# Adding the softmax guard on VectorE instead of ScalarE in a fused attention and mixture-of-experts kernel

## The chip, the cores and the metric

The kernel runs on one core of one Trainium2 chip. The core has TensorE (PE in the profile) for matrix products, VectorE (DVE), ScalarE (ACT) and GpSimd (POOL) for elementwise work, SyncE (SP) and several DMA queues for transfers. The engines run side by side and meet at semaphores: an instruction waits until a counter has reached a value, and raises another one when it is done. The metric is the device time of one execution, in microseconds.

## The reference

Three layers follow one another: attention with rotary embedding, a top-1 mixture of experts, and a dense layer with a tanh. The change lies in attention alone, in the sum that the softmax divides by:

```python
def _attn_ref(q, k, v):                       # (4, 8, 576, 64)
    q_rot, k_rot = (rotate(q), rotate(k))
    scores = scale * np.matmul(q_rot, k_rot.transpose(0, 1, 3, 2))
    scores = scores - np.max(scores, axis=-1, keepdims=True)
    attn = np.exp(scores)
    attn = attn / (np.sum(attn, axis=-1, keepdims=True) + 1e-09)
    return np.matmul(attn, v).astype(np.float32)
```

What comes after it is `_moe_ref` (2304 tokens, 8 experts) and `_moe2_ref` (`g = h - tanh(h)` between two products).

## The kernel before, in words

Attention takes the 32 heads in 16 pairs, 0 to 15. A pair has nine tiles of scores: four of each head with 128 query rows, and one mixed tile of the 64 rows left over from both. The body of pair p runs nine steps, i = 0 to 8, on every engine at once. In a step TensorE computes the scores of tile i of the next pair, p + 1 (L373), transposes a slice of the exponentials of pair p (L420) and multiplies transposed slices with the values (L441, L444, L447). VectorE takes the maximum of the new score tile (`maximum`, L617). ScalarE computes its exponential and the row sums (`exp`, L517). Each transposed slice is then split into a rounded high part, by ScalarE (`round_hi`, L538, `pt_hi`), and the remainder, by VectorE (`split_lo`, L633, `pt_lo`). TensorE multiplies both. So each slice goes TensorE, ScalarE, VectorE, TensorE. The transposed slices of a pair have names; the one of the mixed tile, split in step 5, is M, and the first product that needs both parts of M is that of `values(..., "MA")`, whose first instruction is L441.

GpSimd prepares later pairs: it splits the values (`split_v`, L312 and L317), multiplies the raw q and k with the cosines and sines (`rope`, L338 and L339) and adds and splits the result (`add_up`, L323, L326, L332). These are seven elementwise instructions for each pair, up to pair 12's body. Before the first of them it waits until TensorE is done with the values of the pair before (`pv_done`). SyncE starts the transfers that stack q and k (L184 to L193).

Once a pair, 1e-9 is added to the nine row sums, and the reciprocal is taken. The first is `guard` on ScalarE in step 3 (L548), the second `invert` on VectorE in step 5 (L638). `normalise` uses the reciprocals in the next body. The row sums were finished one body earlier, as `exp` works a pair ahead.

The order on each engine is written out by hand: an engine takes its instructions in the order of the program. Pairs 4 to 13 run on VectorE in a hardware loop, the others are written out; there a semaphore's value has to be computed in a register first.

Of the kernel before, what the change touches and what calls it, by code (L numbers as in the profile page):

```python
# [11 lines left out]
ALU = mybir.AluOpType  # L12
ACT = mybir.ActivationFunctionType
AX = mybir.AxisListType

P = 128
# [26 lines left out]
def attention(nc, qk, v, cos, sin, ident, fold, emb_t, route_consts, x_all, lg_all, tail_dram,  # L43
# [7 lines left out]
    with ExitStack() as ctx:  # L51
        def sb(name, shape, dt=F32):
            return ctx.enter_context(nc.sbuf_tensor(name, shape, dt))

        def sem(name):
            return ctx.enter_context(nc.semaphore(name))
# [3 lines left out]
        TILES = 2 * FULL + 1  # L60
# [26 lines left out]
        neg_max = [sb(f"neg_max{r}", [P, TILES]) for r in range(2)]  # L87
        row_sum = [sb(f"row_sum{r}", [P, TILES]) for r in range(2)]
        guarded = sb("guarded", [P, TILES])
        tiny = sb("tiny", [P, 1])  # L90
        inv_sum = [sb(f"inv_sum{r}", [P, TILES]) for r in range(2)]
        probs = [sb(f"probs{r}", [P, FULL, 2 * S]) for r in range(2)]
        probs_mix = [sb(f"probs_mix{r}", [P, S]) for r in range(2)]
# [28 lines left out]
        zero_set = sem("zero_set")  # L122
# [14 lines left out]
        exp_done = sem("exp_done")  # L137
# [3 lines left out]
        pv_done = sem("pv_done")  # L141
        o_evac = sem("o_evac")
        fold_ready = sem("fold_ready")
        guard_done = sem("guard_done")
        norm_step = sem("norm_step")
        x_done = sem("x_done")
        tail_stored = [sem(f"tail_stored{r}") for r in range(2)]
# [7 lines left out]
        def block_of(i):  # L155

            return i if i < MIX else i - MIX - 1
# [6 lines left out]
        def _(sp):  # L164
# [89 lines left out]

            body(0, 0, first=True)

            sp.wait_ge(zero_set, 2)
            body(1, 1, clears=True)
            with sp.Fori(1, PAIRS // 2 - 2) as m:
                for r in range(2):  # L260
# [249 lines left out]
        @block.scalar  # L510
        def _(act):
            def exp(p, r, i):

                act.wait_ge(max_done, p * TILES + i + 1)
                at = int(i > MIX) * S
                dst = probs_mix[r][:] if i == MIX else probs[r][:, block_of(i), at:at + S]
                nc.scalar.activation(dst, score[(r + i) % 2], ACT.Exp, bias=neg_max[r][:, i:i + 1],  # L517
                                     accum_out=row_sum[r][:, i:i + 1]).then_inc(exp_done, 1)

            def round_hi(p, r, name, first=False):  # L520
                if name[0] == "B":

                    act.wait_ge(pv_done, p * VALUES + VALUE["A" + name[1]] + 1)
                elif not first:
                    last = {"X": "B3", "M": "MB", "C": "MB"}[name] if name in "XMC" else "B" + name[1]

                    act.wait_ge(pv_done, (p - 1) * VALUES + VALUE[last] + 1)

                act.wait_ge(pt_ready, p * UNITS + UNIT[name] + 1)
                src = turned[SLOT[name]]  # L530
                if name == "X":
                    op = nc.scalar.activation(ends[:, 0:FULL, :, 0, :],
                                              src.rearrange("p (k u s) -> p k u s", u=2, s=TAIL), ACT.Identity)
                elif name == "C":
                    op = nc.scalar.activation(ends[:, FULL, :, 0, :], corner.rearrange("p (u s) -> p u s", u=2),
                                              ACT.Identity)
                else:
                    op = nc.scalar.activation(pt_hi[:, FULL if name == "M" else int(name[1]), P:P + MAIN], src,  # L538
                                              ACT.Identity)
                op.then_inc(hi_done, 1)  # L540

            def guard(p, r, first=False):

                act.wait_ge(exp_done, (p + 1) * TILES)
                if not first:

                    act.wait_ge(norm_step, p)
                nc.scalar.activation(guarded[:], row_sum[r][:], ACT.Identity, bias=tiny[:]).then_inc(guard_done, 1)  # L548

            def evac(p, u, first=False):  # L550

                act.wait_ge(pv_done, p * VALUES + VALUE["MB" if u else "MA"] + 1)
                if not first:

                    act.wait_ge(fold_ready, p * 2)
                nc.scalar.activation(out_t[:, u, :], acc, ACT.Identity)
                nc.scalar.activation(out_tail[:, :, u, :], acc_tail[u].rearrange("p (h s) -> p h s", h=2),
                                     ACT.Identity).then_inc(o_evac, 1)

            def body(p, r, first=False, second=False, last=False):  # L560
                for i in range(TILES):
                    round_hi(p, r, STEPS[i][0], first)
                    if i == 1 and not first:
                        evac(p - 1, 1, second)
                    if i == 3:
                        guard(p, r, first)
                    if i == 6:
                        evac(p, 0, first)
                    if not last:
                        exp(p + 1, 1 - r, i)  # L570
                    for name in STEPS[i][1:]:
                        round_hi(p, r, name, first)

            act.dma_start(cos_sb[:, 1, :], cos).then_inc(tables_in, 16)
            act.dma_start(sin_sb[:, 1, :], sin).then_inc(tables_in, 16)
            act.dma_start(id_sb[:], ident).then_inc(consts_in, 16)
            act.dma_start(fold_sb[:, :, E:E + DH], fold.rearrange("p (g d) -> p g d", g=PB)).then_inc(consts_in, 16)
            for u in range(2):
                for w in range(2):
                    act.dma_start(fold_sb[u * DH:(u + 1) * DH, :, w * FW:w * FW + E],  # L580
                                  emb_t.rearrange("(g w d) e -> w d g e", w=2, d=DH)[w]).then_inc(consts_in, 16)

            act.wait_ge(zero_set, 2)
            act.wait_ge(tables_in, 32)
            for table in (cos_sb, sin_sb):
                nc.scalar.activation(table[:, 0, :], table[:, 1, :], ACT.Copy, scale=SCALE).then_inc(table_scaled, 1)
            for i in range(TILES):
                exp(0, 0, i)
            body(0, 0, first=True)
            body(1, 1, second=True)  # L590
            with act.Fori(1, PAIRS // 2 - 1) as m:
                for r in range(2):
                    body(m * 2 + r, r)
            body(PAIRS - 2, 0)
            body(PAIRS - 1, 1, last=True)
            evac(PAIRS - 1, 1)

        @block.vector
        def _(dve):
# [34 lines left out]

            def invert(p, r):

                dve.wait_ge(guard_done, p + 1)
                nc.vector.reciprocal(inv_sum[r][:], guarded[:]).then_inc(norm_step, 1)  # L638

            def normalise(p, r, u, stores=None):  # L640

                dve.wait_ge(norm_step, p + 1)

                dve.wait_ge(fold_ready, p * 2 + u + 1)
                at = u * (MIX + 1)
                by = inv_sum[r][:, at:at + FULL].unsqueeze(2)
                batch, h = p // PB, (p % PB) * 2 + u
                x_at, l_at = E * (1 - u), DH * u
                nc.vector.tensor_tensor(lg_all[:, bass.ds(batch * FULL, FULL), bass.ds(h * E, E)],
                                        folded[1 - u][:, :, l_at:l_at + E], by.to_broadcast([P, FULL, E]), ALU.mult)  # L650
                op = nc.vector.tensor_tensor(x_all[:, bass.ds(batch * FULL, FULL), bass.ds(h * DH, DH)],
                                             folded[1 - u][:, :, x_at:x_at + DH], by.to_broadcast([P, FULL, DH]), ALU.mult)
                if u:
                    if stores is not None:

                        dve.wait_ge(tail_stored[r], stores)
                    op = nc.vector.tensor_tensor(tail_sb[r][:], folded_mix,
                                                 inv_sum[r][:, MIX:MIX + 1].to_broadcast([P, FP]), ALU.mult)
                op.then_inc(x_done, 1)
# [11 lines left out]
                    if i == 3 and not first:  # L671
                        normalise(p - 1, 1 - r, 1, stores)

            nc.vector.memset(tiny[:], 1e-9).then_inc(zero_set, 1)
            nc.vector.memset(zeros[:], 0.0).then_inc(zero_set, 1)
            dve.wait_ge(tables_in, 32)
            rope_first(1, first_k_in, first_k_mult, first_k_done)

# [15 lines left out]
            body(PAIRS - 2, 0, stores=(PAIRS // 2 - 2) * 32)  # L694
            body(PAIRS - 1, 1, last=True, stores=(PAIRS // 2 - 1) * 32)
            normalise(PAIRS - 1, 1, 0)
            normalise(PAIRS - 1, 1, 1, (PAIRS // 2 - 1) * 32)

# [1022 lines left out]
```

## Time and profile before

| | us |
|---|---|
| median of 3 runs | 1111.47 |
| lowest and highest | 1110.96, 1112.81 |
| the profiled execution: its own time | 1110.96 |
| its span in the trace | 1109.1 |
| PE busy | 985.1 (89%) |
| DVE busy | 595.5 (54%) |
| ACT busy | 582.4 (53%) |
| POOL busy | 415.7 (37%) |

Busy times are sums over the whole span, and the stages differ: attention takes the first 350 us or so, and POOL has work mostly there and in the expert layer. An engine can be busy half of the time and still be waited for at one place in each step. A row of the timeline gives an instruction's start and duration in us, and in brackets how long its engine had been idle before it and what ended that.

### The profile page before, as it was taken

How to read it: one execution, taken by the hardware profiler on the slowest of the kernel's cores; microseconds unless marked ns; L12 is line 12 of the kernel's file. 1: busy time of each engine (PE TensorE's matmuls, PEld its weight loads, DVE VectorE, ACT ScalarE, POOL GpSimd, SP SyncE). 2: the span in 40 equal slices, each digit the busy share in tenths (PEclk: the TensorE clock that was granted, in tenths of full speed). 3: DMA queues.
4: the chain of work that ended last, by engine and by line, in shares of the span. 5: the costliest groups of instructions: out<-in, count | busy, mean ns of one | idle time of the engine just before them, and what ended most of it. 6: DMA issues, size and time to landing. Idle time of an engine off the chain costs nothing. (4 is left out here: it accounts for less than half of the span.)

```text
span 1109.1 us, 18954 instructions
## 1 busy us (share of the span) xinstructions
PE 985.1 (89%) x5604; PEld 871.1 (79%) x5605; DVE 595.5 (54%) x1195; ACT 582.4 (53%) x1273; POOL 415.7 (37%) x246
## 2 busy tenths in 40 slices
PE   1899999999995039999999976999999999999996
PEld 1899899989984038888888855888989889899895
DVE  4677777777773731111111104777666666666764
ACT  1677777777772632222322214666565565655653
POOL 3998788887510428309948305000000000000000
PEclk9999999999998569999999997999999999999999
DMA  8777777767503455314433106111000000000001
GB/s 236 192 207 197 219 189 202 206 186 205 145 21 90 169 188 202 97 47 151 152 123 113 38 30 200 58 48 48 1 19 10 0 28 0 13 15 0 28 2 28
DMA packets 63077, 113.82 MB, mean 103 GB/s; under 512 B 20032, under 2 KB 24640, under 8 KB 61120
## 3 DMA queue, kind: packets, MB, share of 16 engines
q1 hardware_dynamic: 52352, 92.62, 29.0%
q10 hardware_dynamic: 7808, 11.31, 3.2%
q0 software_dynamic: 2880, 9.44, 2.5%
q8 instruction: 18, 0.29, 0.1%
q14 instruction: 19, 0.16, 0.1%
HBM read 60.58 MB, written 24.41 MB: 77 GB/s over the span
## 5 line engine op out<-in xcount | busy, mean ns | idle before, releaser
L1429 PE MATMUL hd_ps<-y_hi,w_hi 128*128 128x384 f32 x384 | 130.9, 341 | 7.8 <-DVE g_sb L1599 7.8
L1429 PE MATMUL hd_ps<-y_lo,w_hi 128*128 128x384 f32 x384 | 129.6, 338 | 0.0
L1429 PE MATMUL hd_ps<-y_hi,w_lo 128*128 128x384 f32 x384 | 129.3, 337 | 0.0
L1499 ACT ACTIVATE mag<-hd_ps 128x384 f32<-128x384 f32 x96 | 47.3, 493 | 152.2 <-PE hd_ps L1429 149.8
L617 DVE TENSOR_REDUCE neg_max<-ps 128x1 f32<-128x576 f32 x144 | 108.1, 751 | 31.4 <-PE ps L373 28.9
L633 DVE TENSOR_TENSOR pt_lo<-ps,pt_hi 128x512 fp32r<-128x512 f32 x144 | 99.2, 690 | 43.3 <-ACT pt_hi L538 41.7
L538 ACT ACTIVATE pt_hi<-ps 128x512 fp32r<-128x512 f32 x144 | 86.8, 604 | 58.9 <-PE ps L420 57.5
L1447 PE MATMUL o_ps<-w_hi,g_hi 128*128 128x512 f32 x288 | 115.0, 399 | 2.2 <-DVE g_lo L1608 2.2
L1447 PE MATMUL o_ps<-w_hi,g_lo 128*128 128x512 f32 x288 | 114.3, 397 | 0.0
L1608 DVE TENSOR_TENSOR g_lo<-g_sb,g_hi 128x384 fp32r<-128x384 f32 x96 | 53.5, 558 | 112.3 <-ACT g_hi L1514 112.3
L1447 PE MATMUL o_ps<-w_lo,g_hi 128*128 128x512 f32 x288 | 113.5, 394 | 0.0
L517 ACT ACTIVATE probs<-ps,neg_max 128x576 f32<-128x576 f32 x128 | 95.5, 746 | 26.0 <-DVE neg_max L617 25.7
L420 PE MATMUL ps<-id_sb,probs 128*128 128x128 f32 x576 | 87.8, 279 | 5.4 <-DVE pt_lo L633 5.0
L1102 POOL TENSOR_TENSOR w_hi<-w_stage,one 128x1024 f32 (+1 forms) x32 | 60.6, 1894 | 79.4 <-ACT h_row L1205 59.8
L444 PE MATMUL ps<-pt_hi,v_split 128*128 128x256 f32 (+1 forms) x320 | 85.5, 348 | 1.9 <-issue 0.5
L1429 PEld LDWEIGHTS hd_ps<-y_hi,w_hi 128*128 128x128 f32 x384 | 72.5, 189 | 16.3 <-DVE g_sb L1599 12.9
L373 PE MATMUL ps<-k_hh,q_st 128*128 128x288 f32 x256 | 59.2, 315 | 25.0 <-DMA q_st<-qk_lo 23.1
L1275 DVE TENSOR_TENSOR h_lo<-ht_ps,h_hi 128x512 fp32r<-128x512 f32 x40 | 25.8, 686 | 98.3 <-ACT h_hi L1230 98.3
L1106 POOL TENSOR_TENSOR w_lo<-w_stage,w_hi 128x1024 f32 (+1 forms) x32 | 76.7, 2396 | 4.6 <-POOL w_hi L1102 4.0
L420 PEld LDWEIGHTS ps<-id_sb,probs 128*128 128x128 f32 x576 | 67.7, 142 | 11.2 <-DVE pt_lo L633 9.4
L1429 PEld LDWEIGHTS hd_ps<-y_lo,w_hi 128*128 128x128 f32 x384 | 72.5, 189 | 3.1
L1268 DVE TENSOR_TENSOR x_lo<-xt_ps,x_hi 128x512 fp32r<-128x512 f32 x20 | 13.8, 692 | 110.7 <-ACT x_hi L1213 110.7
(208 smaller groups left out, 2429.8 us busy)
## 6 DMA issues: line engine op xcount, KB each, us to landing
w_stage<-in_w SPq DMA_DIRECT2D x32, 512.0 KB, 3.6
raw_qk<-in_qk SPq DMA_DIRECT2D x14, 1152.0 KB, 6.1
k_hh<-qk_hi SPq DMA_DIRECT2D x64, 144.0 KB, 2.8
k_ll<-qk_lo SPq DMA_DIRECT2D x64, 144.0 KB, 2.9
sorted_rows<-zeros SPq DMA_DIRECT2D x28, 256.0 KB, 6.2
x_row<-sorted_rows ACTq DMA_DIRECT2D x20, 256.0 KB, 2.7
y_rows<-y_row ACTq DMA_DIRECT2D x20, 256.0 KB, 2.1
q_st<-qk_hi SPq DMA_DIRECT2D x32, 144.0 KB, 3.0
```

What stands on the lines that cost most here:

```text
L373: last = nc.tensor.matmul(dst[:, a:z], q_st[r][u][:, at:at + P], keys[r][u][:, key:key + z - a], start=h == 0, stop=h == 1)
L420: last = nc.tensor.transpose(dst[:, j * P:(j + 1) * P], probs[r][:, j, key:key + P], id_sb[:])
L444: nc.tensor.matmul(ps[:, CUT - MAIN // 2 - P + a:CUT - MAIN // 2 - P + z], main, pt_hi[:, k, a:z], start=begin, stop=False)
L517: nc.scalar.activation(dst, score[(r + i) % 2], ACT.Exp, bias=neg_max[r][:, i:i + 1], accum_out=row_sum[r][:, i:i + 1]).then_inc(exp_done, 1)
L538: op = nc.scalar.activation(pt_hi[:, FULL if name == "M" else int(name[1]), P:P + MAIN], src, ACT.Identity)
L617: nc.vector.tensor_reduce(neg_max[r][:, i:i + 1], score[(r + i) % 2], AX.X, ALU.max, negate=True).then_inc(max_done, 1)
L633: nc.vector.tensor_tensor(lo_at, src, hi_at.bitcast(F32), ALU.subtract).then_inc(lo_done, 1)
L1102: nc.gpsimd.tensor_tensor(chunk_of(w_hi, slot, c), stage[:, c % RING, :], one[:].to_broadcast([P, CHUNK]), ALU.mult).then_inc(w_hi_done, 1)
L1106: nc.gpsimd.tensor_tensor(chunk_of(w_lo, slot, c), stage[:, c % RING, :], chunk_of(w_hi, slot, c).bitcast(F32), ALU.subtract).then_inc(w_s ...
L1429: op = nc.tensor.matmul(hd_ps[f % 2][:, 0:G], w[:, c, cols], y[:, c, :], start=c == 0 and h == 0, stop=c == DC - 1 and h == 2)
L1447: op = nc.tensor.matmul(o_ps[:, i, :], a[f % 2][:, rows], w[:, f, :], start=f == 0 and h == 0, stop=f == KF - 1 and h == 2)
L1608: nc.vector.tensor_tensor(g_lo[f % 2][:], g_sb[f % 2][:], g_hi[f % 2][:].bitcast(F32), ALU.subtract).then_inc(glo_done, 1)
```

## The change

The addition of 1e-9 moves from ScalarE to VectorE. The function `guard` is gone, with its semaphore `guard_done`. In `invert` a `tensor_tensor` now adds `row_sum` and `tiny`, and the reciprocal follows behind a wait for it; `norm_step` now goes up twice a pair. `tiny` grows from one column to nine, since it is now a tensor operand of its own and no longer a bias. ScalarE no longer waits for `zero_set` at the start, which now counts to 1.

```diff
-        tiny = sb("tiny", [P, 1])
+        tiny = sb("tiny", [P, TILES])
...
-            sp.wait_ge(zero_set, 2)
+            sp.wait_ge(zero_set, 1)
...
-            def guard(p, r, first=False):
-
-                act.wait_ge(exp_done, (p + 1) * TILES)
-                if not first:
-
-                    act.wait_ge(norm_step, p)
-                nc.scalar.activation(guarded[:], row_sum[r][:], ACT.Identity, bias=tiny[:]).then_inc(guard_done, 1)
-
...
-                    if i == 3:
-                        guard(p, r, first)
...
-            act.wait_ge(zero_set, 2)
             act.wait_ge(tables_in, 32)
...
             def invert(p, r):
 
-                dve.wait_ge(guard_done, p + 1)
+                dve.wait_ge(exp_done, (p + 1) * TILES)
+                nc.vector.tensor_tensor(guarded[:], row_sum[r][:], tiny[:], ALU.add).then_inc(norm_step, 1)
+                dve.wait_ge(norm_step, p * 2 + 1)
                 nc.vector.reciprocal(inv_sum[r][:], guarded[:]).then_inc(norm_step, 1)
 
             def normalise(p, r, u, stores=None):
 
-                dve.wait_ge(norm_step, p + 1)
+                dve.wait_ge(norm_step, p * 2 + 2)
...
-            nc.vector.memset(tiny[:], 1e-9).then_inc(zero_set, 1)
+            nc.vector.memset(tiny[:], 1e-9)
             nc.vector.memset(zeros[:], 0.0).then_inc(zero_set, 1)
+            dve.wait_ge(zero_set, 1)
             dve.wait_ge(tables_in, 32)
```

VectorE in step 5 of the loop's first pair, before. The `neg_max` rows are `maximum`, the `pt_lo` rows `split_lo`; the first `pt_lo` is slice A3 of step 4, the second is M.

```order
L633 TENSOR_TENSOR pt_lo<-ps,pt_hi 128x512 [waits hi_done]
L616 REGISTER_ALU
L617 TENSOR_REDUCE neg_max1<-ps 128x1 [waits scores_ready]
L638 RECIPROCAL inv_sum0<-guarded 128x9 [waits guard_done]
L622 REGISTER_ALU
L633 TENSOR_TENSOR pt_lo<-ps,pt_hi 128x512 [waits hi_done]
```

The same place after the change:

```order
L621 TENSOR_TENSOR pt_lo<-ps,pt_hi 128x512 [waits hi_done]
L604 REGISTER_ALU
L605 TENSOR_REDUCE neg_max1<-ps 128x1 [waits scores_ready]
L626 TENSOR_TENSOR guarded<-row_sum0,tiny 128x9 [waits exp_done]
L627 ISA
L628 RECIPROCAL inv_sum0<-guarded 128x9 [waits norm_step]
L610 REGISTER_ALU
L621 TENSOR_TENSOR pt_lo<-ps,pt_hi 128x512 [waits hi_done]
```

The addition, a register instruction (ISA) and a wait for the addition stand between the maximum of step 5 and the split of M.

ScalarE in step 3 of the same pair, before. The `pt_hi` rows are `round_hi`, the `probs1` row is `exp`.

```order
L538 ACTIVATE pt_hi<-ps 128x512 [waits pt_ready]
L548 ACTIVATE guarded<-row_sum0,tiny 128x9 [waits norm_step,exp_done]
L514 REGISTER_ALU
L517 ACTIVATE probs1,row_sum1<-ps,neg_max1 128x576 [waits max_done]
L529 REGISTER_ALU [waits pv_done]
L535 ACTIVATE pt_hi<-ps 128x2x64 [waits pt_ready]
```

The same place after the change:

```order
L537 ACTIVATE pt_hi<-ps 128x512 [waits pt_ready]
L513 REGISTER_ALU
L516 ACTIVATE probs1,row_sum1<-ps,neg_max1 128x576 [waits max_done]
L528 REGISTER_ALU [waits pv_done]
L534 ACTIVATE pt_hi<-ps 128x2x64 [waits pt_ready]
```

The exponential now follows the rounding directly. On TensorE, GpSimd and SyncE no instruction is added, taken away or moved.

## Rows read from the trace of the kernel before

**Rows 1.** Busy time of each engine in the body of pair 5, us.
```profile
136.00:155.50 19.50, 18.89 (x145) 17.51 (x145) 14.62 (x28) 14.16 (x35) 16.22 (x7) 1.00 0.71 195
```
**Rows 2.** Waits, first 430 us: total us, times, longest us.
```profile
PEld ps L420 <- DVE pt_lo L633: 9.4, 20, 0.6
```
**Rows 3.** Timeline, steps 5 to 7 of pair 5.
```profile
145.43 0.75 DVE L617 TENSOR_REDUCE neg_max<-ps 128x1 f32<-128x576 f32 x1
...
145.69 0.60 ACT L538 ACTIVATE pt_hi<-ps 128x512 fp32r<-128x512 f32 x1 [0.18 <-PE ps L420]
...
146.10 0.20 DVE L638 RECIPROCAL inv_sum<-guarded 128x9 f32<-128x9 f32 x1
...
146.32 0.69 DVE L633 TENSOR_TENSOR pt_lo<-ps,pt_hi 128x512 fp32r<-128x512 f32 x1
...
146.61 0.49 PEld L420 LDWEIGHTS ps<-id_sb,probs 128*128 128x128 f32 x4
...
147.07 0.19 PEld L441 LDWEIGHTS ps<-pt_hi,v_split 128*128 128x128 f32 x1
...
148.03 0.60 ACT L556 ACTIVATE out_t<-ps 128x512 f32<-128x512 f32 x1
```
**Rows 4.** Timeline of ScalarE, step 3 of pair 5.
```profile
140.85 0.29 ACT L548 ACTIVATE guarded<-row_sum,tiny 128x9 f32<-128x9 f32 x1
...
141.04 0.73 ACT L517 ACTIVATE probs<-ps,neg_max 128x576 f32<-128x576 f32 x1
...
142.54 0.28 ACT L535 ACTIVATE pt_hi<-ps 128x128 fp32r<-128x128 f32 x1 [0.68 <-PE ps L412]
```
**Rows 5.** Timeline, GpSimd around `invert`: pair 5, then pairs 2, 11, 12.
```profile
146.03 2.67 POOL L323 TENSOR_TENSOR rotated<-by_cos,by_sin 128x1152 f32<-128x1152 f32 x1
...
148.65 2.66 POOL L326 TENSOR_TENSOR qk_hi<-by_cos,by_sin 128x1152 fp32r<-128x1152 f32 x1
...
87.66 2.67 POOL L323 TENSOR_TENSOR rotated<-by_cos,by_sin 128x1152 f32<-128x1152 f32 x1
...
87.80 0.20 DVE L638 RECIPROCAL inv_sum<-guarded 128x9 f32<-128x9 f32 x1
...
262.30 2.68 POOL L323 TENSOR_TENSOR rotated<-by_cos,by_sin 128x1152 f32<-128x1152 f32 x1
...
262.34 0.20 DVE L638 RECIPROCAL inv_sum<-guarded 128x9 f32<-128x9 f32 x1
...
281.60 2.68 POOL L323 TENSOR_TENSOR rotated<-by_cos,by_sin 128x1152 f32<-128x1152 f32 x1
...
281.77 0.20 DVE L638 RECIPROCAL inv_sum<-guarded 128x9 f32<-128x9 f32 x1
```
**Rows 6.** Timeline, GpSimd around `invert` in pair 0.
```profile
47.00 2.67 POOL L338 TENSOR_TENSOR by_cos<-raw_qk,cos_sb 128x1152 f32<-128x1152 f32 x1
...
49.28 0.20 DVE L638 RECIPROCAL inv_sum<-guarded 128x9 f32<-128x9 f32 x1
```
**Rows 7.** Timeline of VectorE, two small additions or products, the second dependent.
```profile
360.55 0.17 DVE L888 TENSOR_TENSOR emb_n<-emb_n 128x8 f32<-128x8 f32 x1
360.75 0.17 DVE L889 TENSOR_TENSOR emb_n<-emb_n 128x8 f32<-128x8 f32 x1
```
**Rows 8.** Timeline of the routing stage, VectorE and GpSimd.
```profile
384.35 1.23 DVE L1001 TENSOR_TENSOR w_lo<-w_stage,w_hi 128x1024 f32 x1 [0.76 <-ACT w_hi L859]
...
384.72 1.68 POOL L832 DMA_INDIRECT sorted_rows<-token_rows,pos_i  x1 [0.30 <-issue]
...
389.46 1.27 DVE L1001 TENSOR_TENSOR w_lo<-w_stage,w_hi 128x1024 f32 x1 [1.12 <-ACT w_hi L859]
...
389.47 0.96 POOL L832 DMA_INDIRECT sorted_rows<-token_rows,pos_i  x1 [0.31 <-issue]
```
**Rows 9.** Timeline of the start, VectorE and SyncE's queue.
```profile
13.91 0.76 DVE L611 TENSOR_TENSOR qk_lo<-probs,qk_hi 128x576 fp32r<-128x576 f32 x1
...
15.32 1.30 SPq L193 DMA_DIRECT2D q_st<-qk_hi  x2
```

More of the change, by code:

```diff
@@ L143, in attention @@
         fold_ready = sem("fold_ready")
-        guard_done = sem("guard_done")
         norm_step = sem("norm_step")
```

## The prediction

> **What bounds the kernel now.** I read the busy times by stretch first. The body of pair 5 is a fair sample of attention: in 19.50 us TensorE is busy for 18.89, VectorE 14.62, ScalarE 14.16 and GpSimd 16.22, at a granted clock of 1.00 [rows 1]. TensorE sets the pace, the others have 3 to 5 us of slack each on average. That average hides how the engines meet, so the waits come next: TensorE's weight loads of the transposes wait for VectorE's `pt_lo` 20 times, 9.4 us in all and never more than 0.6 [rows 2]. TensorE therefore does wait for VectorE at times. The last view, the timeline around `invert`, shows how tight it is at the very place of the change [rows 3]. ScalarE's high part of M ends at 145.69 + 0.60 = 146.29, and VectorE's split of M starts at 146.32, 0.03 later. The split ends at 147.01, and TensorE's first load of `values("MA")` starts at 147.07. The load before it, a group of four, began at 146.61 and ran 0.49, to 147.10, with a little overlap as usual, so TensorE arrives there at the same moment. The slack between this split and TensorE is about 0.01 us. VectorE itself arrives a bit early: the reciprocal starts at 146.10 and overlaps its successor, as the maximum (145.43 + 0.75 = 146.18) overlapped the reciprocal by 0.08, so the split could start at 146.22 and waits 0.10 for ScalarE.
>
> Hence a delay d of VectorE between the maximum of step 5 and the split of M costs d - 0.10 - 0.01 there. It isn't made up later in the body: ScalarE's `evac` at 148.03 [rows 3] waits for the product with M, and the exponential and the roundings behind it on ScalarE move with it, and TensorE waits for those roundings' slices.
>
> **The change part by part.** *ScalarE loses the guard.* It starts at 140.85, and the exponential behind it at 141.04: the guard holds ScalarE's queue for 0.19 us, 16 times, 3.0 us in all [rows 4]. Behind that exponential ScalarE is idle for 0.68 us until TensorE has transposed the small corner [rows 4]. The 0.19 us only lengthens that idle time. Value: 0; if the cover were gone, a gain of 3.0.
>
> *The start.* ScalarE no longer waits for two memsets that were over long before, and its table load stands ahead of the wait for the tables. Even if this lets VectorE finish q earlier, SyncE starts q's stacking at 15.32, while VectorE's last part is done at 13.91 + 0.76 = 14.67 [rows 9]: SyncE is 0.65 us late by itself, busy with k's eight transfers. Value: 0, for `zero_set`, the wider `tiny` and VectorE's wait for its own memset too. If the cover were gone it would be some tenths once, either way.
>
> *VectorE gains an addition and a wait for it,* while nothing else stands in the way. A small `tensor_tensor` takes 0.17 us, and one that depends on it starts 0.20 after it [rows 7]. So the reciprocal starts 0.20 later than now, and the split can follow at 0.20 + 0.20 - 0.08 = 0.32 after the addition's start, where now it follows at 0.22 [rows 3]. That is 0.10 a pair, less 0.01 slack. In the loop a register instruction is added, which may cost up to another 0.1 or nothing. This hits 15 pairs (in pair 15 no scores are computed and VectorE has slack): 1.4 us, between 0 and 3.
>
> *The addition meets GpSimd.* It is the first VectorE instruction inside attention's steady state that reads two SBUF tensors (`row_sum` and `tiny`); the maxima read PSUM alone, `split_lo` and `normalise` PSUM and one SBUF tensor, the reciprocal one. At this moment GpSimd is in a long instruction that reads SBUF. In pair 5 its L323 started at 146.03, 0.07 us ahead of VectorE at 146.10, and the next one, L326, starts at 148.65 [rows 3, 5]. It is so in each of the eleven pairs 2 to 12: L323 starts 0.14 ahead in pair 2, 0.04 in pair 11, the closest, and 0.17 in pair 12 [rows 5]. The distance is stable because both engines follow TensorE's `pv_done` of the same product by fixed chains.
>
> Whether the two can read at once, the trace of before shows only from the side. In the routing stage VectorE runs a subtraction of two SBUF tensors from 384.35 to 385.58. GpSimd's indirect DMA issued at 384.72 takes 1.68 us, where the one at 389.47 takes 0.96 [rows 8]. It is longer by 0.72, nearly the 0.86 us for which VectorE's subtraction was still running: it waited for it. At 389.46 both start within 0.01; GpSimd takes its usual time and VectorE 1.27 instead of 1.23 [rows 8]. So there is something that one has to give up before the other gets it, and whoever comes second waits. The other order, VectorE behind a long elementwise GpSimd instruction, appears nowhere. Its bounds: 0.04 us (the one time VectorE was stretched) and the remainder of GpSimd's instruction, or that and one more. I take the remainder, as the row where one came clearly second waited for nearly all of it. L323 lasts until the next instruction at +2.62, less the 0.11 that VectorE comes behind on average over the eleven pairs: a wait of 2.51. With the 0.10 from above and the 0.01 of slack it is 2.60 a pair, 28.6 us for eleven.
>
> The Trainium skill says this outright ("SBUF — State Buffer", section "Who interferes with whom"): a VectorE instruction with two SBUF inputs contends with a GpSimd instruction that reads SBUF, and the one that comes second waits until the first has ended. By that rule the sum is the one that I make here; by the stretched row of VectorE alone it would be 0.04 a pair, some 2 us in all. Of the direction that counts, VectorE behind GpSimd's elementwise work, no row here speaks.
>
> *The other pairs.* In pair 0 GpSimd's L338 runs until 49.67 and VectorE comes at 49.28 [rows 6]: 0.39 + 0.09, about 0.5. In pair 1 GpSimd isn't tied to TensorE yet and both have been shifted by pair 0; anything from 0.1 to 2.7, and I take 0.5, as in pair 0. In pairs 13 and 14 GpSimd has no work left: 0.1 each. Pair 15: 0. Together 1.2.
>
> *Knock-on.* GpSimd has 3.3 us of idle time a pair [rows 1], and a longer body gives it more room. TensorE idles for 2.5 us in 22, at a clock of 1.00 now; I price no loss of clock.
>
> **Sum.** 28.6 + 1.2 = 29.8 us on the profiled execution's own 1110.96, 1140.8. The median before is 0.5 above that execution: 1141.3, I say 1141.
>
> **Rivals.** *A, the forecast:* every pair from 2 to 12 waits out L323: 1135 to 1148, the width being pair 1 (2 us), the register instruction (1 us) and a release up to 0.3 us earlier or later in each of eleven pairs (3 us). 0.62.
>
> *B, only some pairs wait.* The distance is 0.04 to 0.17 us and alternates: about 0.15 in the even pairs, about 0.05 in the odd. If GpSimd takes what it needs a little after its recorded start, the six even pairs wait and the five odd ones slip in between L339 and L323. Then 6 x 2.55 + 5 x 0.1 + 1.2 = 17, 1128. For it: the closeness. Against it: at 389.46 and 389.47 GpSimd, with the later recorded start, was not held up [rows 8]. 0.18.
>
> *C, GpSimd's next instruction goes first again.* L326 follows L323 without a gap; if it doesn't let VectorE in, the wait is 2.62 longer: 29.8 + 11 x 2.62 = 58.6, 1170. Against it: VectorE has been waiting for longer than L326. 0.07.
>
> *D, elementwise GpSimd work holds nothing up.* Only the addition's own cost stays: 1.4, at most 3: 1113. For it: VectorE was stretched by 0.04 at most. Against it: rows 8 in the other order. 0.09.
>
> *E, faster.* ScalarE's 0.19 us counts: it decides if the exponential behind the guard is awaited in its step, by `maximum` or a transpose, and VectorE's addition fits into the 0.10 that it now waits for M's high part. Then up to 3.0 less, 1108.5. Against it: the idle 0.68 behind that exponential [rows 4]. 0.04.
>
> **How the numbers follow.** About 0.2%, 2.2 us, is what a measurement can tell from no change. A, B and C are slower beyond it, 0.87, and a third of D, 0.03: 0.90. The rest of D: same 0.06. E: faster 0.04. The predicted time is A's. The range reaches from B's lower side to past A, 1120 to 1152, and holds A and B, 0.80; below lie D and E, above it C.
>
> **What the profile afterwards would show.** Right: in the eleven pairs the addition (or an idle stretch or a long duration of it) takes VectorE some 2.5 us, ending when L326 starts; behind it TensorE's L441 shows a wait for `pt_lo` of about 2.6 us that isn't there now; bodies of pairs 2 to 12 take 22 us instead of 19.4 (from 262.34 to 281.77 [rows 5]), those of pairs 13 and 14 no more than 0.2 longer; ScalarE's idle time before L535 grows by 0.2. The stages behind attention keep their length. Wrong: an addition of 0.17 us next to a running L323 (D); bodies of 22 and 19.5 us by turns (B); a wait over two GpSimd instructions (C); or, the other way round, L323 delayed by the addition because VectorE gets there first.

## The result

| | before | after |
|---|---|---|
| median us (4 runs each) | 1111.28 | 1142.25 |
| lowest to highest | 1110.96 to 1112.81 | 1141.73 to 1142.58 |
| the profiled execution: its own time | 1110.96 | 1142.72 |
| span in the trace | 1109.1 | 1140.9 |

The ratio is 1.0275, interval 1.0257 to 1.0293: slower by 31 us. The forecast was 1141.

### The profile page after: what moved, and what is told of

Read it like the earlier page. It is cut to its first block and busy times, and to the rows that moved or that the text cites. A ratio compares the mean times of both kernels' runs of the same rounds, so it can differ in the third digit from the quotient of the medians.

```text
span 1140.9 us, 18958 instructions
## 1 busy us (share of the span) xinstructions
PE 993.9 (87%) x5604; PEld 881.5 (77%) x5605; DVE 624.4 (55%) x1211; ACT 580.4 (51%) x1257; POOL 415.8 (36%) x246
## 3 DMA queue, kind: packets, MB, share of 16 engines
q1 hardware_dynamic: 52352, 92.62, 28.2%
## 5 line engine op out<-in xcount | busy, mean ns | idle before, releaser
L419 PE MATMUL ps<-id_sb,probs 128*128 128x128 f32 x576 | 91.1, 289 | 4.0 <-DVE pt_lo L621 3.7
L443 PE MATMUL ps<-pt_hi,v_split 128*128 128x256 f32 (+1 forms) x320 | 87.8, 356 | 2.3 <-DVE pt_hi L621 0.9
L419 PEld LDWEIGHTS ps<-id_sb,probs 128*128 128x128 f32 x576 | 72.6, 148 | 7.2 <-DVE pt_lo L621 6.2
```

The source lines that it names most:

```text
L419: last = nc.tensor.transpose(dst[:, j * P:(j + 1) * P], probs[r][:, j, key:key + P], id_sb[:])
L443: nc.tensor.matmul(ps[:, CUT - MAIN // 2 - P + a:CUT - MAIN // 2 - P + z], main, pt_hi[:, k, a:z], start=begin, stop=False)
```

## The profile after

A stretch of one body's length beside that of [rows 1], from just after the split of M in pair 4 to just after the one in pair 5 (us, then busy us and count of PE, PEld, DVE, ACT, POOL, granted clock, DMA share, GB/s):

```profile
136.00:158.40 22.40, 20.09 (x146) 19.23 (x146) 17.00 (x28) 14.17 (x33) 16.19 (x8) 0.92 0.59 155
```

The stretch is 2.9 us longer than before. VectorE's busy time grew by 2.4 us, though it only got an addition of nine columns; ScalarE and GpSimd did no more than before. The mean clock is 0.92 and no longer 1.00.

The waits of attention that have grown (first 430 us: total us, times, longest us), and the addition's 16 executions (duration in ns, min, median, max):

```profile
PEld ps L440 <- DVE pt_lo L621: 28.2, 14, 2.5
ACT out_t L547 <- PE ps L446: 31.6, 15, 2.6
L626 DVE TENSOR_TENSOR guarded<-row_sum,tiny x16: 158/2524/2611, 48.5 to 366.7; 128x9 f32<-128x9 f32 x16
```

TensorE now waits for the split of M 28.2 us in all, where the trace of before has such a wait only once, 0.5 us in pair 15, and ScalarE's `evac` waits for TensorE behind that (2.8 us, twice, before). The addition takes 0.16 us in pairs 13 to 15, where GpSimd has no work, 2.52 to 2.61 in pairs 2 to 12, and 0.48 and 0.79 in pairs 0 and 1. The same place as in [rows 3], timeline of all engines:

```profile
153.88 0.75 DVE L605 TENSOR_REDUCE neg_max<-ps 128x1 f32<-128x576 f32 x1
...
154.50 2.63 POOL L322 TENSOR_TENSOR rotated<-by_cos,by_sin 128x1152 f32<-128x1152 f32 x1
...
154.54 2.61 DVE L626 TENSOR_TENSOR guarded<-row_sum,tiny 128x9 f32<-128x9 f32 x1
...
155.05 0.49 PEld L419 LDWEIGHTS ps<-id_sb,probs 128*128 128x128 f32 x4
...
157.09 2.65 POOL L325 TENSOR_TENSOR qk_hi<-by_cos,by_sin 128x1152 fp32r<-128x1152 f32 x1
...
157.19 0.22 DVE L628 RECIPROCAL inv_sum<-guarded 128x9 f32<-128x9 f32 x1
157.32 0.66 DVE L621 TENSOR_TENSOR pt_lo<-ps,pt_hi 128x512 fp32r<-128x512 f32 x1
...
158.03 0.19 PEld L440 LDWEIGHTS ps<-pt_hi,v_split 128*128 128x128 f32 x1 [2.48 <-DVE pt_lo L621]
...
159.00 0.60 ACT L547 ACTIVATE out_t<-ps 128x512 f32<-128x512 f32 x1 [2.58 <-PE ps L446]
```

GpSimd starts 0.04 us ahead of VectorE (0.07 in this pair before). The addition is shown as running for the whole of GpSimd's instruction, and ends at 157.15, 0.06 us after the next one's recorded start; the blocked VectorE instruction shows as busy, not idle. TensorE loads the weights of the last transposes at 155.05, and then no weights for 2.48 us.

The distance from one reciprocal to the next shows the second part of the loss. Pairs 10, 11 and 12, VectorE:

```profile
267.57 0.21 DVE L628 RECIPROCAL inv_sum<-guarded 128x9 f32<-128x9 f32 x1
...
289.96 0.22 DVE L628 RECIPROCAL inv_sum<-guarded 128x9 f32<-128x9 f32 x1
...
311.83 0.21 DVE L628 RECIPROCAL inv_sum<-guarded 128x9 f32<-128x9 f32 x1
```

22.39 and 21.87 us, where the same two distances were about 19.4 (262.34 to 281.77 in [rows 5]): every second one is 0.5 longer still. Windows of pairs 4 and 5 show why:

```profile
134.00:136.00 2.00, 0.37 (x3) 0.37 (x4) 1.97 (x4) 0.11 (x1) 2.00 (x2) 1.00 0.83 276
136.00:140.00 4.00, 4.00 (x22) 3.98 (x22) 2.29 (x4) 3.13 (x8) 1.33 (x1) 0.57 0.78 265
140.00:156.00 16.00, 15.73 (x124) 14.88 (x122) 12.35 (x21) 10.61 (x26) 12.46 (x6) 1.00 0.54 132
```

From 134 to 136 lies most of the stop behind pair 4's addition: TensorE is busy for 0.37 of 2 us. From 136.5 for 3.4 us its granted clock is 1.2 GHz instead of 2.4 (0.57 over the four us), and TensorE is busy without a gap, only slower. There are six such stretches in attention after the change, from 92.1, 136.5, 180.9, 225.2, 269.6 and 314.0, and none before it; the trace of before, all of attention's bodies at once:

```profile
50.00:335.00 285.00, 276.23 (x2118) 258.69 (x2117) 210.12 (x380) 208.29 (x499) 211.03 (x92) 1.00 0.65 176
```

## The experiments

The runs stand in three groups, each beside its own runs of the kernel before: 1111.23 us for e1 to e4, 1115.83 for e5 to e7, 1116.34 for e8 and e9. Where a diff leaves lines out, `...` stands for them. In the second and third group the ratio is the number to read; 1111.3 times the ratio puts it on the scale of the first.

**One input instead of two (e1_reduce).** Row sum and 1e-9 lie side by side and are added by a reduction.

```diff
-        row_sum = [sb(f"row_sum{r}", [P, TILES]) for r in range(2)]
+        pair_sum = [sb(f"pair_sum{r}", [P, TILES, 2]) for r in range(2)]
+        row_sum = [t[:, :, 0] for t in pair_sum]
...
-                nc.vector.tensor_tensor(guarded[:], row_sum[r][:], tiny[:], ALU.add).then_inc(norm_step, 1)
+                nc.vector.tensor_reduce(guarded[:], pair_sum[r][:], AX.X, ALU.add).then_inc(norm_step, 1)
...
             nc.vector.memset(tiny[:], 1e-9)
+            for r in range(2):
+                nc.vector.memset(pair_sum[r][:, :, 1], 1e-9)
```

> The changed kernel with one edit: the addition is done by a tensor_reduce over pairs (row sum, 1e-9) that lie side by side in one SBUF tensor, so VectorE reads one SBUF tensor instead of two. Same place, same number of instructions and waits. Port theory (two SBUF inputs collide with GpSimd's reads): the instruction takes 0.16 to 0.2 us in every pair, bodies last 19.4 to 19.5 us, 1110 to 1114 us, no low clock inside attention. Rival (the additional instruction with its wait for its own semaphore, or ScalarE's lost guard, makes the loss): stays at 1142.

1111.69 us, ratio 1.0006 (0.9997 to 1.0015). Pair 5, GpSimd and VectorE, and the addition's line:

```profile
146.36 2.67 POOL L323 TENSOR_TENSOR rotated<-by_cos,by_sin 128x1152 f32<-128x1152 f32 x1
...
146.40 0.16 DVE L627 TENSOR_REDUCE guarded<-pair_sum 128x9 f32<-128x18 f32 x1
146.60 0.22 DVE L629 RECIPROCAL inv_sum<-guarded 128x9 f32<-128x9 f32 x1
146.73 0.66 DVE L622 TENSOR_TENSOR pt_lo<-ps,pt_hi 128x512 fp32r<-128x512 f32 x1
...
L627 DVE TENSOR_REDUCE guarded<-pair_sum x16: 161/163/164, 49.5 to 337.1; 128x9 f32<-128x18 f32 x16
```

It comes 0.04 us behind GpSimd as in the changed kernel, and takes 0.16 in all 16 pairs. The additional instruction, its wait and ScalarE's lost guard together cost nothing that the times can tell. The whole loss hangs on the form of the addition; two things differ in it, the second SBUF input and the kind of instruction, and the next run takes them apart.

**An immediate (e2_imm).**

```diff
-                nc.vector.tensor_tensor(guarded[:], row_sum[r][:], tiny[:], ALU.add).then_inc(norm_step, 1)
+                nc.vector.tensor_scalar(guarded[:], row_sum[r][:], 1e-9, None, ALU.add).then_inc(norm_step, 1)
```

> The changed kernel with the addition as a tensor_scalar with an immediate: one SBUF tensor, 9 columns. Theory 'two SBUF tensors' as the traces have shown it so far: 0.16 to 0.2 us, 1110 to 1114. Rival: a tensor_scalar also needs what GpSimd holds, since it may read one tensor over both ports, then it waits like the tensor_tensor, 2.5 us in eleven pairs, 1139 to 1143. The Trainium skill (SBUF - State Buffer, Who interferes with whom) says that tensor_scalar can enter such a mode, and speaks for the rival.

1143.03 us, ratio 1.0292 (1.0273 to 1.0311): the rival held. Pair 5, and then pair 1:

```profile
155.47 2.64 POOL L322 TENSOR_TENSOR rotated<-by_cos,by_sin 128x1152 f32<-128x1152 f32 x1
...
155.53 2.61 DVE L626 TENSOR_SCALAR guarded<-row_sum 128x9 f32<-128x9 f32 x1
```

```profile
69.31 0.16 DVE L626 TENSOR_SCALAR guarded<-row_sum 128x9 f32<-128x9 f32 x1
...
69.32 2.68 POOL L322 TENSOR_TENSOR rotated<-by_cos,by_sin 128x1152 f32<-128x1152 f32 x1
```

A `tensor_scalar` with one SBUF tensor waits like the `tensor_tensor`, so "two SBUF tensors" is too narrow. The Trainium skill ("SBUF — State Buffer", section "Who interferes with whom") says that a `tensor_scalar`, where its operands allow it, can enter a mode in which it contends with GpSimd for the ports that the two share. The trace agrees, with 2.61 us here in pair 5. In pair 1 VectorE's record starts 0.01 us ahead of GpSimd's, and it doesn't wait.

**Another phase (e3_early).** `invert` stands ahead of the maximum of step 5.

```diff
                 for i in range(TILES):
+                    if i == 5:
+                        invert(p, r)
                     if not last:
                         maximum(p + 1, 1 - r, i)
...
-                    if i == 5:
-                        invert(p, r)
```

> The changed kernel with invert one instruction earlier, ahead of the maximum of step 5, some 0.66 us earlier. Theory (VectorE waits for the end of the GpSimd instruction that is running when it comes): it meets the last 0.6 us of L338 instead of the whole of L322, the addition takes 0.5 to 0.7 us in the eleven pairs, but maximum and split both stand behind it: 0.4 to 0.6 us a pair, 1115 to 1120. Rival A (the length of the wait doesn't depend on the phase): 2.5 us and 1142. Rival B (GpSimd's next instruction goes first): 3.2 us a pair, 1148 to 1150.

1118.14 us, ratio 1.0064 (1.0046 to 1.0083). Pair 5:

```profile
145.33 2.66 POOL L338 TENSOR_TENSOR by_sin<-raw_qk,sin_sb 128x1152 f32<-128x1152 f32 x1
148.06 2.65 POOL L322 TENSOR_TENSOR rotated<-by_cos,by_sin 128x1152 f32<-128x1152 f32 x1
```

```profile
147.46 0.56 DVE L626 TENSOR_TENSOR guarded<-row_sum,tiny 128x9 f32<-128x9 f32 x1
148.05 0.21 DVE L628 RECIPROCAL inv_sum<-guarded 128x9 f32<-128x9 f32 x1
```

The addition waits only for the rest of the instruction that is running, and is through before the next starts. Bodies last 19.8 us, 0.4 more than before. Nearly four fifths of the loss are gone by moving two instructions by 0.66 us.

**At the front of the body (e4_front).** The same edit with `i == 0`.

> The changed kernel with invert as the first thing in each body, ahead of the maximum of step 0, where GpSimd has no work and VectorE idles for about a us before the change. Theory: the addition with two SBUF tensors takes 0.16 us from pair 2 on, nothing waits, 1109 to 1112, the same as before or up to 1 us faster since the reciprocal leaves the tight place. Rival (the two-input addition is slow wherever it stands next to GpSimd's stream, or leaving ScalarE costs): above 1130.

1112.03 us, ratio 1.0011 (1.0002 to 1.0020). The time came out at the upper edge of what I expected, 0.1% slower and not faster. The expectation of the addition was wrong:

```profile
L626 DVE TENSOR_TENSOR guarded<-row_sum,tiny x16: 169/584/2520, 37.9 to 330.0; 128x9 f32<-128x9 f32 x16
```

GpSimd's last instruction of the body, L331, is still running there, and the addition waits 0.4 us for it from pair 2 on (1.1 in pair 1, and 2.3 for L325 in pair 0). Before the change VectorE was idle ahead of this maximum for 1.2 us a body (14.1 us in twelve), and that absorbs the wait: bodies last 19.36 and 19.39. So a wait of 0.4 us costs nothing here and all of itself in e3_early's place.

**The collision alone (e5_extra).** The kernel before, guard on ScalarE, with one addition more that nobody waits for.

```diff
+        extra_in = sb("extra_in", [P, TILES])
+        extra = sb("extra", [P, TILES])
...
+                nc.vector.tensor_tensor(extra[:], extra_in[:], extra_in[:], ALU.add)
                 dve.wait_ge(guard_done, p + 1)
                 nc.vector.reciprocal(inv_sum[r][:], guarded[:]).then_inc(norm_step, 1)
...
+            nc.vector.memset(extra_in[:], 1.0)
...
+            dve.wait_ge(zero_set, 2)
```

> The kernel before, guard still on ScalarE, with one more VectorE instruction ahead of the reciprocal: an addition of two SBUF tensors of 9 columns whose result nobody reads and nobody waits for. Port theory: it alone brings the loss, 2.4 us in eleven pairs and the low-clock stretches, 1136 to 1142; a little less than the change since nothing waits for its result. Rival (moving the guard off ScalarE or the wait for the own semaphore matters): 1112 to 1114.

1145.94 beside 1115.83, ratio 1.0284 (1.0254 to 1.0314); the change's 1.0275 lies inside. On the first scale it is 1142.9, a little above the range that I expected. Pair 5, VectorE, and the line over all pairs:

```profile
153.60 2.61 DVE L639 TENSOR_TENSOR extra<-extra_in 128x9 f32<-128x9 f32 x1
156.13 0.20 DVE L641 RECIPROCAL inv_sum<-guarded 128x9 f32<-128x9 f32 x1
...
L639 DVE TENSOR_TENSOR extra<-extra_in x16: 159/2531/2606, 48.6 to 363.7; 128x9 f32<-128x9 f32 x16
```

Nobody waits for the result, and still everything behind it on VectorE stands still until it is through. In pairs 0 and 1 the addition comes just ahead of GpSimd's next instruction and takes 0.16 us.

**Only the even pairs (e7_even).** The tiles are those of e1_reduce.

```diff
...
-                nc.vector.tensor_tensor(guarded[:], row_sum[r][:], tiny[:], ALU.add).then_inc(norm_step, 1)
+                if r:
+                    op = nc.vector.tensor_reduce(guarded[:], pair_sum[r][:], AX.X, ALU.add)
+                else:
+                    op = nc.vector.tensor_tensor(guarded[:], row_sum[r], tiny[:], ALU.add)
+                op.then_inc(norm_step, 1)
```

> The changed kernel with the two-input addition in the even pairs only (six of the eleven that wait); the odd pairs use the tensor_reduce over one tensor. Each wait costs 2.45 us without a change of clock, from the odd-to-even distances of the changed kernel (21.87 against 19.4), so 14.7 us. Theory 1: the clock falls only where such a wait comes in every body; no low stretch, 1126 to 1128. Theory 2: the wait of an even pair alone brings the 3.4 us stretch at half clock and 0.6 us each, 1129 to 1131.

1131.7 beside 1115.83, ratio 1.0165 (1.0125 to 1.0204), which is 1125 to 1134 on the first scale and doesn't decide. The trace shows something between the two theories: six long additions (median 2.51 us) but two low stretches, behind those of pairs 10 and 12 only. The window around pair 10's:

```profile
253.00:257.20 4.20, 2.02 (x16) 1.78 (x15) 4.17 (x5) 1.36 (x4) 4.20 (x2) 1.00 0.59 155
257.20:261.20 4.00, 4.00 (x23) 3.99 (x22) 2.40 (x5) 3.07 (x8) 0.70 (x2) 0.57 0.80 274
```

Here the prices come apart. Without a low stretch the reciprocals are 19.40 apart where no wait lies between them and 21.86 where one does (172.75, 192.15, 214.01); with a low stretch and no wait it is 19.95 (255.27, 275.22). Against 19.35 and 19.43 before, a wait costs 2.4 to 2.5 us and a low stretch 0.55.

**GpSimd only writes (e6_memset).** L322's addition becomes a memset, ahead of its wait. This kernel leaves out the sum that belongs in `rotated`, so what follows attention gets other data; only attention's bodies are compared.

```diff
-                pool.wait_ge(mult_done, k + 1)
-                nc.gpsimd.tensor_tensor(rotated[:], by_cos[:], by_sin[:], ALU.add)
+                nc.gpsimd.memset(rotated[:], 0.0)
+                pool.wait_ge(mult_done, k + 1)
```

> The changed kernel with GpSimd's L322 (by_cos + by_sin into rotated) replaced by a memset of rotated to zero, which writes SBUF and reads nothing; the lower part of q and k is then wrong and the routing behind attention gets other data, so only attention's bodies are compared. Theory (it is GpSimd's reading that collides): the addition meets the memset and takes 0.16 us, bodies of 19.4 us. Rival (any GpSimd instruction blocks): the addition lasts until the memset's end, 1 us or more.

Pair 5, and then pair 0, where the addition still meets a multiplication:

```profile
147.55 1.05 POOL L321 MEMSET rotated<- 128x1152 f32 x1
148.57 2.66 POOL L325 TENSOR_TENSOR qk_hi<-by_cos,by_sin 128x1152 fp32r<-128x1152 f32 x1
```

```profile
147.73 0.16 DVE L626 TENSOR_TENSOR guarded<-row_sum,tiny 128x9 f32<-128x9 f32 x1
```

```profile
48.40 2.65 POOL L338 TENSOR_TENSOR by_sin<-raw_qk,sin_sb 128x1152 f32<-128x1152 f32 x1
```

```profile
48.95 2.12 DVE L626 TENSOR_TENSOR guarded<-row_sum,tiny 128x9 f32<-128x9 f32 x1
```

Inside the running memset the addition takes 0.16 us, and bodies last 19.4 to 19.5; in pair 0 of the same run it waits for the multiplication to the end. So the two-input addition collides with GpSimd's reading, and not with its writing. For the `tensor_scalar` of e2_imm no run tells the two apart.

**VectorE late without a collision (e9_busy).** The kernel before, with work of VectorE's own.

```diff
+        extra = sb("extra", [P, 2])
...
                     if i == 5:
+                        if not last:
+                            for j, table in enumerate((cos_sb, sin_sb)):
+                                nc.vector.tensor_reduce(extra[:, j:j + 1], table[:].rearrange("p b s -> p (b s)"), AX.X, ALU.max)
                         invert(p, r)
```

> The kernel before, guard on ScalarE, with two maxima over one SBUF tensor of 1152 columns each (cosines, sines; results unused) on VectorE ahead of the reciprocal, in the 15 bodies that compute scores: 2 x 1.27 = 2.5 us of VectorE's own work, one SBUF input, no collision with GpSimd. Theory (TensorE loses whatever VectorE is late in the tight place, 0.11 us less, whoever makes it late, and the clock falls after such stops): 15 x 2.4 = 36 us and 7 or 8 low stretches of 0.57 us, 1149 to 1153; GpSimd's L323 and the next stay 2.63 apart. Rival (it is the collision itself that costs beyond the lateness, in the clock or on GpSimd): no low stretch, 1146 to 1148.

1154.87 beside 1116.34, ratio 1.0329 (1.0302 to 1.0356), which is 1148 on the first scale, 1 below the expected range. Pair 5, VectorE:

```profile
158.83 1.34 DVE L671 TENSOR_REDUCE extra<-cos_sb 128x1 f32<-128x1152 f32 x1
160.09 1.34 DVE L671 TENSOR_REDUCE extra<-sin_sb 128x1 f32<-128x1152 f32 x1
161.35 0.20 DVE L639 RECIPROCAL inv_sum<-guarded 128x9 f32<-128x9 f32 x1
161.47 0.63 DVE L634 TENSOR_TENSOR pt_lo<-ps,pt_hi 128x512 fp32r<-128x512 f32 x1
```

The reciprocal is 2.52 us late, bodies without a low stretch last 21.6 to 21.8, that is 2.3 longer, and there are seven low stretches. So neither TensorE's loss behind a late VectorE nor the clock needs the collision; that only makes VectorE late. The passing on is a little short of complete: 2.3 of 2.5, where I had expected 2.4. The split of M has a part in that: it takes 0.63 us here and 0.69 in [rows 3].

**Both cures (e8_front_reduce).** e1_reduce with `invert` at the front of the body.

> Both cures at once: the addition as a reduction over one SBUF tensor, and invert at the front of the body, ahead of the maximum of step 0. Nothing of the guard is left on ScalarE or in step 5. Theory: the reciprocal was never what the split of M waited for (ScalarE was), so bodies keep 19.4 us, 1109 to 1112, no gain beyond 0.1%. Rival (the reciprocal's place counts): 0.05 to 0.1 us a body, 1109.5 or less. The additions take 0.16 us, where e4_front's took 0.55 to 0.61.

1116.96 beside 1116.34, ratio 0.9999 (0.9987 to 1.0012). The additions take 0.17 us, the distance of reciprocals from pair 3 on is 19.33 to 19.35 and 19.42 to 19.47 in turn. No version beats the kernel before, which fits that the split of M waited for ScalarE there and not for the reciprocal.

## Why the prediction was right

*TensorE has no slack at the split of M:* right. The wait of 2.48 us stands at L440, and e9_busy shows that it doesn't matter what made VectorE late.

*ScalarE's guard and the start are worth nothing:* right for ScalarE. e1_reduce has no guard there and is no faster, and e5_extra has it and is as slow as the change. At the start the traces differ by more than any such effect: the first addition starts at 48.45 in the changed kernel and at 49.86 in e2_imm, which has the same code there, so nothing is to be read from that.

*The addition and its wait, 0.10 a pair:* a little too high. In e1_reduce the distances are 19.41 and 19.51, against 19.35 and 19.43: 0.06 and 0.08, or 0.05 over all bodies of pairs 0 to 12 (233.10 instead of 232.49 us in twelve). The split starts 0.33 us after the addition (146.40 to 146.73), as forecast (0.32). But it takes 0.66 us there instead of the 0.69 of [rows 3], and so ends only 0.07 later, which the forecast left out.

*The addition waits out L323 in pairs 2 to 12:* right in all eleven, and the term was sized well but not exactly. I took 2.51 for the wait and 0.17 for the addition, 2.68; the rows show 2.52 and 2.61 in turn, 2.56, since it is finished 0.06 us after GpSimd's next recorded start (0.02 ahead of it in pair 2). If its own 0.16 us come last, it was let in about 0.1 us before that start. From pair 1's reciprocal to pair 12's the trace has 242.95 us (68.88 to 311.83) instead of 213.24 (68.53 to 281.77), 29.7 more, and 27.0 without the five low stretches in between: 2.45 for each of eleven waits instead of 2.60, 27.0 instead of 28.6.

*Pairs 0, 1, 13 and 14, 1.2 us:* 1.0, that is 0.3 in pair 0 and 0.6 in pair 1 by the addition's durations there (0.48 and 0.79 against 0.16), and 0.1 for the others.

*No loss of clock:* wrong. Six stretches of 3.4 us at half clock, 0.55 each, cost 3.3 us. I saw the stop of TensorE coming and priced only its length. Why so long a stretch at half the clock costs no more than 0.55 the runs don't show.

Sum by the runs: 27.0 + 1.0 + 3.3 = 31.3, of a span longer by 31.8; 1140.8 was forecast for an execution that took 1142.72. From pair 0's reciprocal to pair 15's the trace is 31.1 us longer. Behind that it is 774.0 us instead of 773.0; e2_imm has 772.6 and e1_reduce 773.4 with the same code there, so I read nothing from this. The mechanism was right, but that the total came out so close is partly luck: a term too large by 1.6 and the missing 3.3 partly cancel.

*The rivals.* B (some pairs slip in before GpSimd) was not so in pairs 2 to 12: even 0.04 us behind is behind. But the closeness was real: in e2_imm's pair 1 VectorE was 0.01 us ahead and went first. C (GpSimd's next instruction goes first) and D are out by the rows above, E by e1_reduce and e8_front_reduce.

## What to carry to other kernels

Before moving a small operation to VectorE next to a busy GpSimd, look at its form and its SBUF inputs, and see what GpSimd is doing at that moment: nine columns cost 2.5 us a time here because GpSimd was 0.04 to 0.14 us ahead with an instruction of 2.6 that reads SBUF. The cure is in the operand (a reduction over one tensor, 0.16 us) or in the place (where VectorE idles), and an immediate instead of the second tensor is no cure. Look in the timeline for small instructions with a duration that GpSimd's rows explain; the wait shows as busy time. A stop of TensorE has a price beyond its length if the granted clock falls behind it.

## What the runs showed of the hardware that I had not expected

- TensorE's granted clock fell to 1.2 GHz for 3.4 us behind some of its 2.5 us stops, six times with eleven stops in a row (five in e5_extra), seven times with fifteen (e9_busy), and twice where they came in every second body (e7_even); each cost 0.55 us in the changed kernel. Stops that came with e3_early's additions of 0.5 us brought none. Which stops are followed by one I can't tell; it stays open.
- A `tensor_scalar` with an immediate, 9 columns of fp32 in SBUF, waits for GpSimd's `tensor_tensor`: 2.53 and 2.61 us in turn. A `tensor_reduce` of 18 columns and a reciprocal of 9 at the same place don't.
- VectorE's wait ends about 0.1 us before the recorded start of GpSimd's next instruction, an estimate from ends 0.06 behind that start and a length of 0.16. GpSimd's instructions follow each other without a gap there, and in none of eleven pairs did VectorE wait for a second one. In pair 0 of e5_extra the addition came 0.09 us ahead of that start, with GpSimd's L340 still recorded as running, and didn't wait:

```profile
46.11 2.66 POOL L340 TENSOR_TENSOR by_cos<-raw_qk,cos_sb 128x1152 f32<-128x1152 f32 x1
48.74 2.66 POOL L341 TENSOR_TENSOR by_sin<-raw_qk,sin_sb 128x1152 f32<-128x1152 f32 x1
```

```profile
48.65 0.16 DVE L639 TENSOR_TENSOR extra<-extra_in 128x9 f32<-128x9 f32 x1
```
